# Later keys and queries loaded in 32 by 32 squares and transposed by VectorE, in a fused attention and two-layer kernel

## The reference

```python
def _attn_ref(q, k, v):
    B, H, S, D = q.shape                     # 4, 8, 576, 64
    q_d = q.reshape(B, H, S // 4, 4, D).mean(axis=3)      # k_d, v_d likewise
    out_d = sm_attn(q_d, k_d, v_d)                        # softmax attention of the means
    mask = np.abs(pos[:, None] - pos[None, :]) < 4
    scores = np.where(mask, scale * q @ k^T, -1e9)
    out_local = softmax(scores) @ v
    return np.repeat(out_d, 4, axis=2) + out_local

def _moe_ref(x, g_ln, w_ch1, w_ch2):         # 512 -> 2048 -> 512
    xn = (x - mu) / np.sqrt(var + 1e-06) * g_ln
    return x + np.maximum(xn @ w_ch1, 0.0) @ w_ch2

def _moe2_ref(x, mu_k, mu_r, w_k, w_v, w_r): # shift by one position, mix, 512 -> 1024 -> 512, gate
    k = np.maximum(xk @ w_k, 0.0)
    return sigmoid(xr @ w_r) * (k * k @ w_v)
```

## Time and profile before

| | |
|---|---|
| median of 3 runs | 835.48 us (833.46 to 835.61) |
| the profiled execution | 833.43 us, of which the span of instructions is 831.5 us |
| TensorE busy | 803.3 us, 97% |
| VectorE, ScalarE, GpSimd busy | 436.9, 305.2, 263.6 us |
| turns in unit 0 and later | 144 transposes of 96x128, from 85.0 to 449.0 us |
| DMA | 80401 packets, 47.93 MB, mean 58 GB/s |
| mean granted clock of TensorE | 0.981 |

### The profile page before, as it was taken

One profiled execution on the slowest core, in us unless ns is written; L12 is line 12 of the kernel. 1 busy time (PEld: TensorE's weight loads), 2 busy tenths in 40 slices (PEclk: granted clock), 3 DMA queues, 4 the chain that ended last, 5 costly groups with the idle time before them and its releaser, 6 DMA issues.

```text
span 831.5 us, 14604 instructions
## 1 busy us (share of the span) xinstructions
PE 803.3 (97%) x5976; PEld 732.8 (88%) x5976; DVE 436.9 (53%) x716; ACT 305.2 (37%) x680; POOL 263.6 (32%) x274
## 2 busy tenths in 40 slices
PE   4879999999999999999999999999999999999998
PEld 3768999999999999999999999999788888888886
DVE  5468645433543524534543353265677757575654
ACT  5664533233332323332323322154543433333322
POOL 4455763314543423354431442201211111111111
PEclk9589999999999999999999999999999999999999
DMA  9960440010152011043000000451202002001010
GB/s 172 288 209 2 94 81 30 21 40 30 30 125 50 2 41 49 1 98 62 30 19 14 29 12 1 159 175 51 79 1 102 1 0 77 1 6 46 1 51 25
DMA packets 80401, 47.93 MB, mean 58 GB/s; under 512 B 60112, under 2 KB 69328, under 8 KB 80336
## 3 DMA queue, kind: packets, MB, share of 16 engines
q1 hardware_dynamic: 80336, 47.01, 21.1%
HBM read 37.57 MB, written 9.44 MB: 57 GB/s over the span
## 4 chain that ended last, share of the span: by engine, by line
PE 89%; DVE 3%; POOL 2%; issue 2%; ACT 2%; DMA 1%; POOLq 0%; SPq 0%; ACTq 0%; DVEq 0%
PE psY L902 24%; PE psH L885 24%; PE psY L955 11%; PE psH L936 11%; PE psA L918 6%; PE psA L791 2%; PE psA L818 2%; PE psA L804 2%; PE psA L739 1%; PE psA L777 1%; PE psA L750 1%; DMA v_raw<-in_v_dram 1%; PE psA L763 1%; DVE prob L1311 1%; DVE mixin L1419 1%
## 5 line engine op out<-in xcount | busy, mean ns | idle before, releaser
L1467 DVE SCALAR_TENSOR_TENSOR h_lo<-psH,h_hi 128x288 fp32r<-128x288 f32 x128 | 58.1, 454 | 228.2 <-ACT h_hi L1236 228.0
L902 PE MATMUL psY<-h_hi,w_hi 128*128 128x288 f32 x512 | 161.2, 315 | 0.0
L885 PE MATMUL psH<-xc_hi,w_hi 128*128 128x288 f32 x512 | 157.3, 307 | 2.4 <-DVE xc_lo L1358 2.4
L885 PE MATMUL psH<-xc_hi,w_lo 128*128 128x288 f32 x512 | 151.9, 297 | 0.0
L902 PE MATMUL psY<-h_lo,w_hi 128*128 128x288 f32 x512 | 151.0, 295 | 0.0
L902 PE MATMUL psY<-h_hi,w_lo 128*128 128x288 f32 x512 | 151.0, 295 | 0.0
L885 PE MATMUL psH<-xc_lo,w_hi 128*128 128x288 f32 x512 | 150.6, 294 | 0.0
L1236 ACT ACTIVATE h_hi<-psH 128x288 fp32r<-128x288 f32 x128 | 52.5, 410 | 208.3 <-PE psH L885 208.1
L724 POOL TENSOR_TENSOR relu_k<-relu_k 128x512 f32<-128x512 f32 (+1 forms) x40 | 38.7, 966 | 252.4 <-ACT relu_k L1195 252.4
L902 PEld LDWEIGHTS psY<-h_hi,w_hi 128*128 128x128 f32 x512 | 96.5, 188 | 6.9 <-issue 2.5
L885 PEld LDWEIGHTS psH<-xc_hi,w_hi 128*128 128x128 f32 x512 | 96.8, 189 | 4.8 <-issue 2.7
(11 more groups left out here) (173 smaller groups left out, 1492.5 us busy)
## 6 DMA issues: line engine op xcount, KB each, us to landing
w_raw<-in_moe_w_ch_dram SPq DMA_DIRECT2D x8, 1024.0 KB, 9.0
x_scratch<-x SPq DMA_DIRECT2D x8, 576.0 KB, 3.4
out_dram<-gate SPq DMA_DIRECT2D x18, 256.0 KB, 2.2
raw<-in_q_dram SPq DMA_DIRECT2D x21, 192.0 KB, 4.4
v_raw<-in_v_dram SPq DMA_DIRECT2D x12, 288.0 KB
raw<-in_k_dram SPq DMA_DIRECT2D x18, 192.0 KB, 3.2
x_sh<-x_scratch SPq DMA_DIRECT2D x3, 1026.0 KB, 5.6
v_win<-in_v_dram SPq DMA_DIRECT2D x14, 208.0 KB
```

Of the source, the lines that this page charges most:

```text
L885: ins = mm(psH[:, m % 2, 0:N], ws[a][:, kt, f * P:(f + 1) * P], xx[bb][:, kt], start=(kt == 0 and i == 0), stop=(kt == KT - 1 and i == 2))
L902: ins = mm(psY[:, d, 0:N], ws[a][:, f, d * P:(d + 1) * P], hs[bb][:, m % 2], start=(f == 0 and i == 0), stop=(f == NF1 - 1 and i == 2))
L1467: nc.vector.scalar_tensor_tensor(out=h_lo[:, m % 2], in0=psH[:, m % 2, 0:N], scalar=0.0, in1=h_hi[:, m % 2].bitcast(F32), op0=ALU.max, op1 ...
```

## The change

Only the first unit's keys and queries are still turned by TensorE. For all later ones `raw` gets another shape, 3 places of 128 partitions by 2 by 288. A load (`load_later`) now covers half of the 512 features of 288 positions. It is 8 DMAs, one for each 32 partitions and each of two feature blocks; each has 32 partitions with 9 runs of 128 bytes, so that a square of 32 positions by 32 features lies where its transpose belongs. VectorE transposes within the squares with one instruction of 128x576 (`flip`), writes `kT` or `qT` directly, and sums the groups one slot later (`sum_flipped`), or, for unit 1, after both flips. The flips stand first in their slot. The table `FLIPS` puts them 18, 16, 14, 12 (keys), 10 and 7 (queries) slots ahead of the unit in which their attention is done, which are slots 14, 16, 18, 20, 22 and 25 of the unit before. There are 26 of them: 4 for the keys of units 2, 4 and 6, and 2 for the queries of units 1 to 7. The copies of ScalarE for these turns are gone. At the start, the first three loads move behind the pieces `load_w2(0)` and `load_w1(1)`, and two more follow at the place where three did.

```diff
-LATER = [(-17, "Tk", 0), (-14, "Tk", 1), (-11, "Tk", 2), (-9, "Tq", 0), (-6, "Tq", 1), (2, "Sd", 0), (4, "Sd", 1),
+LATER = [(2, "Sd", 0), (4, "Sd", 1),
...
+    SQ = 32
+    HALF = KT // 2
+    FLIPS = [(-18, "k", 0, 0), (-16, "k", 0, 1), (-14, "k", 1, 0), (-12, "k", 1, 1), (-10, "q", 0, 0), (-7, "q", 0, 1)]
...
-        raw = sb(ctx, "raw", [P, RAW, E])
+        raw = sb(ctx, "raw", [P, RAW, HALF, N])
...
             def load_later(j):
+                what, u, c, i = flips[j]
                 if j >= RAW:
-                    sp.wait_ge(turned, chunks[j - RAW][3] + 1)
-                load_chunk(*chunks[j][0:3], raw[0:W, j % RAW], raw_in[j % RAW])
+                    sp.wait_ge(flipped, j - RAW + 1)
+                t0 = (c if what == "k" else u % 2) * N
+                for a in range(P // SQ):
+                    head, d0 = a * SQ // D, a * SQ % D
+                    for jj in range(HALF):
+                        src = (k if what == "k" else q)[u // 2, (P // D) * (HALF * i + jj) + head, t0:t0 + N, d0:d0 + SQ]
+                        sp.dma_start(raw[a * SQ:(a + 1) * SQ, j % RAW, jj].rearrange("t (y d) -> t y d", d=SQ),
+                                     src.rearrange("(y t) d -> t y d", t=SQ)).then_inc(raw_in[j % RAW], 16)
...
             load_w1(0)
+            load_w2(0)
+            load_w1(1)
             for j in range(RAW):
                 load_later(j)
-            load_w2(0)
-            load_w1(1)
...
-            for j in range(RAW):
+            for j in range(HALF):
                 load_later(j + RAW)
...
+            def flip(what, u, c, i):
+                at = flip_of[what, u, c, i]
+                dst = (kT if what == "k" else qT)[:, HALF * i:HALF * (i + 1), c * N:(c + 1) * N]
+                dve.wait_ge(raw_in[at % RAW], 16 * (P // SQ) * HALF * (at // RAW + 1))
+                dve.wait_ge(s_done, WIN_B * (u // 2) if what == "k" else NW_U * u)
+                nc.vector.transpose(dst, raw[:, at % RAW]).then_inc(flipped, 1)
+
+            def sum_flipped(what, u, c, i):
+                src, dst = (kT, kdT) if what == "k" else (qT, qdT)
+                dve.wait_ge(flipped, flip_of[what, u, c, i] + 1)
+                dve.wait_ge(sd_done, 2 * u)
+                group_sum(src[:, HALF * i:HALF * (i + 1)], dst[:, HALF * i:HALF * (i + 1)], c * GU, GU)
...
             def attend(slot):
+                for x_ in flips_at(slot):
+                    flip(*x_)
+                for x_ in flips_at(slot - 1):
+                    if flip_of[x_] >= HALF:
+                        sum_flipped(*x_)
                 for what, u, n in work_at(DVE_WORK, slot):
```

More of the change, by code:

```diff
@@ L79, in fused_kernel @@
     for u in range(1, NU):
-        later += [(SLOTS * (u - 1) + s, kind, u, n) for s, kind, n in LATER if (kind != "Tk" or u % 2 == 0) and (kind, u) != ("Tq", 1)]
+        later += [(SLOTS * (u - 1) + s, kind, u, n) for s, kind, n in LATER]
     for u in range(NU):
@@ L87, in fused_kernel, with flips_at, flipped_by @@
     turn_of = {x: i for i, x in enumerate(turns)}
-    N_TURN0 = sum(u == 0 for _, u, _ in turns)
-    chunks = [(what, u, c, i) for i, (what, u, n) in enumerate(turns) if u for c in TURN[what][n]]
+    N_TURN0 = len(turns)
+    SQ = 32
+    HALF = KT // 2
+    FLIPS = [(-18, "k", 0, 0), (-16, "k", 0, 1), (-14, "k", 1, 0), (-12, "k", 1, 1), (-10, "q", 0, 0), (-7, "q", 0, 1)]
+    flips_by_slot = [(SLOTS * (u - 1) + s, what, u, c, i) for u in range(1, NU) for s, what, c, i in FLIPS
+                     if what == "q" or u % 2 == 0]
+    flips = [x[1:] for x in flips_by_slot]
+    flip_of = {x: i for i, x in enumerate(flips)}
     RAW = 3
+    def flips_at(slot):
+        return [x[1:] for x in flips_by_slot if x[0] == slot]
+    def flipped_by(u):
+        return flip_of["q", u, 0, 1] + 1
     def pair_at(i):
@@ L399, in coarse, with turn_source @@
             return tile[0:GU, 0:4 * SD].rearrange("p (a j c) -> p a j c", a=2, c=SD)
[L401 to L414, removed]
+        def turn_source(what, n, x):
+            return (k_first if what == "Tk" else q_first)[0:W, TURN[what][n][x]]
         def vw_slot(w):
@@ L549, in _ @@
             load_v_sum(1, 0)
-            for j in range(RAW):
+            for j in range(HALF):
                 load_later(j + RAW)
             for slot in range(-LEAD, SLOTS * NU):
+                for x_ in flips_at(slot):
+                    if HALF <= flip_of[x_] < len(flips) - RAW:
+                        load_later(flip_of[x_] + RAW)
                 for kind, u, n in steps_at(slot):
[L554 to L557, removed]
                     if kind == "AV" and NW_U * u + n + 2 < NWIN:
@@ L730, in _, with turn @@
             mm = nc.tensor.matmul
-            def turn(what, u, n):
-                i = place_of[what, u, n]
-                wait_turn_in(pe, what, u, n)
+            def turn(what, n):
+                i = place_of[what, 0, n]
+                pe.wait_ge(first_in[turn_of[what, 0, n]], 16 * len(TURN[what][n]))
                 wait_bank_out(pe, i)
                 for x in range(len(TURN[what][n])):
-                    src = turn_source(what, u, n, x)
+                    src = turn_source(what, n, x)
                     for j in range(KT):
@@ L848, in attend @@
                 for kind, u, n in steps_at(slot):
[L849 to L851 removed]
+                    if kind == "Sd":
                         scores_d(u, n)
@@ L1134, in attend @@
                 for what, u, n in work_at(ACT_WORK, slot):
[L1135 to L1139, removed]
+                    if what == "exp_d":
                         exp_d(u, n)
@@ L1388, in attend @@
             def attend(slot):
-                for what, u, n in work_at(DVE_WORK, slot):
-                    if what == "sum_k":
-                        group_sum("Tk", u, n)
-                    elif what == "sum_q":
-                        group_sum("Tq", u, n)
-                    elif what == "top_d":
+                for x_ in flips_at(slot):
+                    flip(*x_)
+                for x_ in flips_at(slot - 1):
+                    if flip_of[x_] >= HALF:
+                        sum_flipped(*x_)
+                for what, u, n in work_at(DVE_WORK, slot):
+                    if what == "top_d":
                         top_of_d(u, n)
@@ L1459, in _ @@
             lo_x(0)
-            group_sum("Tq", 1, 0)
-            group_sum("Tq", 1, 1)
+            for i in range(HALF):
+                flip("q", 1, 0, i)
+            for i in range(HALF):
+                sum_flipped("q", 1, 0, i)
             dve.wait_ge(params_in, 48)
```

91 lines of the change are left out of this document (39 added, 52 removed), and 2 rows, old and new, of the table FIRST.

## The result

The changed kernel takes 845.35 us (median of four runs, 844.82 to 847.08); the kernel before took 834.92 us in the same comparison (833.46 to 835.61). The ratio is 1.013, 95% interval 1.011 to 1.015: slower by 10.4 us, where I had forecast 5.3 us less. The profiled execution has a span of 843.0 us against 831.5.

What follows compares the result with a forecast made beforehand. TensorE, busy 97%, was taken as the bound, beside GpSimd's chain to `mean`. +1.1 (unit 0) - 2.2 - 2.2 (units 2, 4) - 3.2 (odd units) + 1.2 (v_raw) = -5.3 us: 833.43 to 828.1 us, range 823.0 to 839.0.

Steps and rivals of the forecast that it cites:

- rival 3: DMA queue: small packets or issues cost double, 5.4 us a load, delaying v_raw, `mean` and the start; 851 us; chance 0.17 with milder forms.
- the one on SyncE: SyncE and DMA queue: eight issues per load take 2.4 to 4 us, covered by 4.2 us for two slots.
- 0.2 us for each of the two v_raw loads: DMA queue ahead of `mean` in three units: v_raw sharing it with raw loads costs 1.2 us in all.
- issues of 0.3 us: SyncE: sign expected in the profile after, the time one DMA issue takes.
- 0.9 us in each of units 2 and 4: `mean` on TensorE: wait for GpSimd's chain, cutting the 3.1 us gain to 2.2 us in each unit.
- v_raw takes over 5 us to land: DMA queue: one of the signs that would show the forecast wrong.
- my 13.9: DMA queue: ns per packet of 128 bytes, from a line through two packet sizes; 2.0 us a load.
- The 12.5 us removed: TensorE's main loop: 144 transposes go, 3.1 us in each even unit, 1.05 us in each odd one.
- rival 2: VectorE: a flip takes 1.5 us, making x later in units 0, 2 and 4; 834.1 us; chance 0.13.
- Unit 0's x, 1.8 us late: VectorE in unit 0: two flips and a sum ahead of x delay GpSimd's chain; unit net 1.1 us slower.
- rival 4: Kernel start: 16 issues over 0.75 us each bring a weight piece some 3 to 6 us late; 834 us; chance 0.08.
- Rival 1: Whole kernel: the cover holds everywhere and all 12.5 us come in; 823.0 us; chance 0.12 with mixtures.

Runs made afterwards that it cites:

- run 2: Changed kernel with each raw-load DMA cut into two halves of 16 partitions (416 DMAs for 208, same packets): 886.34 us.
- run 4: Changed kernel with SyncE issuing each raw load two slots behind the flip that frees its place: 832.85 us, ratio 0.996.
- run 9: Changed kernel with raw loads issued two slots later, sums of v in slots 17, 23, 29, 37, flips and their sums at slot end: 824.88 us, ratio 0.988.
- run 1: Changed kernel with all flips kept but raw loads after the first three left out: 829.17 us, ratio 0.991.
- run 3: Kernel before with its later chunk loads cut into four DMAs each (156 for 39, packets of 256 bytes): 835.93 us, ratio 0.999.
- run 5: Changed kernel with GpSimd's sums of v moved from slots 17, 19, 21, 23 to 17, 23, 27, 30: 835.29 us, ratio 0.998.
- run 7: Changed kernel with raw loads issued two slots later and sums of v in slots 17, 23, 34, 37: 828.98 us, ratio 0.991.
- run 10: Changed kernel with raw loads issued two slots later, sums of v in slots 17, 23, 29, 37, flips at slot head: 826.29 us, ratio 0.990.
- run 8: Changed kernel with raw loads issued two slots later and flips and their sums at slot end, behind x: 831.41 us, ratio 0.993.

## Why the prediction was wrong

The forecast's sign was wrong and the time lies outside of the range. The kernel lost by rival 3's way, v_raw late and `mean` waiting for it, in a milder form and for a cause that I had dismissed.

**The step that failed** is the one on SyncE: "8 are 2.4 to 4 us, within 4.2 us for two slots", and "At 2.0 to 2.7 us a load these are drained; I count 0.2 us for each of the two v_raw loads". The issues cost 4.0 us, my own upper end, but I compared one group with two slots and never laid the sequence out in time. The rows had a median of 0.53 us already, that is 4.2 us for eight; my list of signs even said "issues of 0.3 us". Between the flip of slot 14 and the sum there are 7.5 us, and two groups and a `v_win` take 9.1. I had reckoned a load by its queue time (2.0 to 2.7 us) and put the issues down as covered. Instead of 0.9 us in each of units 2 and 4 and 0.4 us of v_raw in each even unit, `mean` waits 12.7 us. The 0.2 us a load was wrong as well: the loads of unit 2 take 5.7 and 4.3 us for 3.8 and 3.5, and my own sign, "v_raw takes over 5 us to land", came true. Runs 2 and 4 show the cause from both sides: with twice the issues `mean` waits 9.6 us more (of 41 us in all); with the same issues two slots later it waits 7.6 us less, and the time falls by 12.5 us. In run 4 a load still takes 4.1 to 4.7 us; what makes that stays open.

**A term that was missing** is the clock. I counted a wait at its own length. Behind the waits of 3.9 to 4.8 us TensorE came back at the lower level: 2.3, 1.5 and 1.2 us at `mean`, and about 1 us behind the wait for x. The trace of before had no such wait in the main loop, but its first stretches did show half speed. That is some 6 us of the 16.8 between the forecast of the span (831.5 - 5.3) and the span (843.0).

**Rival 3** had the right place with the wrong cause. It wanted packets of over 24 ns. Measured in the changed kernel, in a stretch with nothing but these loads:

```profile
229.00:235.00 6.00, 6.00 (x59) 5.71 (x58) 3.00 (x7) 1.31 (x3) 4.24 (x5) 1.00 0.39 62
```

0.39 of 6 us and 16 engines, over 62 GB/s x 6 us / 128 bytes = 2906 packets: 12.9 ns against my 13.9. The queue is busy for 39% of that stretch while SyncE issues without a pause. The Trainium skill, "DMA: Bandwidth & Descriptors", Why small descriptors are slow, gives 11 cycles to a packet of 256 bytes, and counted its way one of 128 has 7 (my estimate), a ratio of 0.64; the rows give 12.9 / 18.6 = 0.69, near enough. The same page's rule of 512 bytes or more (Specifications) speaks of a cost that didn't decide here.

**Right, by steps.** The 12.5 us removed: odd units are 1.04 to 1.06 us shorter, for 1.05 forecast, and run 9 brings units 2 and 4 down by 3.15 and 3.12. The flip, 0.75 us taken; the tile view of the changed kernel:

```profile
L1274 DVE STREAM_TRANSPOSE kT<-raw x12: 765/768/770, 87.9 to 378.5; 128x576 f32<-128x576 f32 x12
```

So rival 2 falls. The Trainium skill's one element per cycle and lane ("Vector Engine (DVE) Microarchitecture Reference", The reshape front-end and per-opcode configuration) agrees with it; the estimate of 1.4 us scaled from its 2-byte transposes doesn't. Unit 0's x, 1.8 us late: it starts at 93.52 against 89.78, and of these 3.7 us the start of the kernel makes 1.7, so 2.1 (TensorE's wait, 3.41 us, is in the waits above). The start: the first of three weight pieces goes out at 57.54, not at the 52 I had, since ten microseconds pass over 16 issues in a full queue, yet ScalarE doesn't wait for it (its first use is at 64.27). So rival 4 falls for the changed kernel, by a margin that run 2 uses up: there the piece goes out at 72.30 and ScalarE waits 13.8 us. Rival 1, all 12.5 us, isn't the changed kernel's, but run 9 comes within 2 us of it. And the rest of the sum: without the v_raw trouble units 2 and 4 gain 2.9 and 2.7 us in run 1, for 2.2 forecast; the 0.9 us at `mean` was too pessimistic.

**Not shown to be the change.** TensorE reaches full pitch at about 50 us in the profiled execution of before, at 56.7 in that of after, read from the starts of its matmuls (in run 3 the granted clock of the rows says 1.00 there, at half the pitch). Run 3, whose TensorE program is that of before, has 56.6, and runs 1 and 4, with the changed start, 50.4 and 49.7. It varies between executions of either start, and costs about 1.6 us. It is late in eight of the ten profiled executions with the changed start and in two of four with the old one; too few to say whether the start has a part in it.

## What to carry to other kernels

Before splitting a load into n DMAs, write out what the issuing engine does between the moment at which each single-buffered load behind it may go and its turn: here 0.5 us an issue, at 36 KB as at 18, so two groups of eight held back the issue of v_raw by 1.7 us and all of a chain with it. The repair is order and not speed: issue what somebody is waiting for first, and the prefetch, which has slots to spare, behind it. And a new wait of TensorE is to be priced with the slow matmuls that may follow it: 1.2 to 2.3 us behind waits of 3.9 to 4.8 us here.

## What the runs showed of the hardware that I had not expected

- Halving a DMA of 32 partitions x 9 runs of 128 bytes leaves its issue at 0.51 us (0.50 before); DMAs of v_raw, larger in bytes (288 KB), take 0.31 us.
- A VectorE operation of 72x4 took 1.24 instead of 0.17 us beside GpSimd's addition of two tiles, and ended with it (129.89 + 1.24 = 131.13, 129.82 + 1.28 = 131.10). The Trainium skill, "SBUF — State Buffer", Terms, says that the two engines share a port pair that one of them holds for a whole instruction; the rows agree, and 1.0 us in each of three units was the price.
- The length of a wait doesn't tell whether the clock falls behind it. After the wait of 3.4 us for x the granted clock was 0.66 to 0.79 over the stretch from 93 to 98 us in the changed kernel and runs 4, 5, 7 and 10, and 0.50, then 0.83, in run 1. After the same wait of 1.9 us for x it stayed at 1.00 in run 8 and fell to 0.66 in run 9, and behind one of 1.8 us near 57 us it fell in run 1 and not in run 4. What decides that, these runs leave open. Runs 8 and 9 in that stretch:

```profile
93.00:98.00 5.00, 5.00 (x51) 4.72 (x50) 3.20 (x4) 2.33 (x4) 4.84 (x6) 1.00 0.29 61
```
```profile
93.00:98.00 5.00, 5.00 (x31) 4.84 (x31) 2.43 (x4) 2.33 (x4) 4.46 (x5) 0.66 0.30 58
```

- Open too: why v_raw takes 4.1 to 6.0 us to land beside raw loads and 3.5 and 3.6 us without them (run 1, unit 4), and with that the 2 us by which run 4 missed.
